# A second square per chunk taken in halves, its GpSimd work rearranged, and a VectorE order turned round, in a fused attention and two-layer kernel on one core

## The reference

```
x  = softmax(q k^T / sqrt(128)) k            # 768 pooled keys
h1 = x @ w_in1;  g1 = relu(h1)**2;  x2 = g1 @ w_out1          # 2048 wide
h  = x2 @ w_in2                                               # 2048 wide
g2 = (a0 + a1 h + a2 h^2 + a3 h^3) / (1 + |b0||h| + |b1|h^2 + 1e-6)
out = g2 @ w_out2
```

## Time and profile before

| | |
|---|---|
| time, median of 3 runs | 1517.82 us (1517.7 to 1518.0) |
| time of the profiled execution | 1517.89 us |
| its span | 1515.9 us |
| PE busy | 1483.7 us (98%) |
| DVE busy | 1445.2 us (95%) |
| ACT busy | 1378.8 us (91%) |
| POOL busy | 1248.3 us (82%) |
| granted TensorE clock | full throughout |

### The profile page before, as it was taken

The page is one execution under the profiler, slowest core; times in us unless marked ns, Lnnn a source line. Parts: engine busy times, 40 slices in busy tenths (PEclk is TensorE's granted clock), DMA queues, the critical chain, the costliest instruction groups (busy, mean ns, idle before and its releaser), DMA issues.

```text
span 1515.9 us, 20584 instructions
## 1 busy us (share of the span) xinstructions
PE 1483.7 (98%) x5576; PEld 991.1 (65%) x5576; DVE 1445.2 (95%) x2549; ACT 1378.8 (91%) x2672; POOL 1248.3 (82%) x1225
## 2 busy tenths in 40 slices
PE   5999999999999999999999999999999999999988
PEld 4999999765666666666666666666666666666655
DVE  7888888889999999999999999999999999999998
ACT  3777777689999999999999999999999999999997
POOL 4544445359999999999999999999999999999897
PEclk9999999999999999999999999999999999999999
DMA  6200001000000000000000000000000000000000
GB/s 224 84 21 28 21 27 43 1 1 1 8 8 8 1 8 8 8 8 1 7 8 8 0 8 8 8 1 8 7 8 1 8 8 8 8 1 8 8 8 7
DMA packets 11518, 24.21 MB, mean 16 GB/s; under 512 B 1440, under 2 KB 2336, under 8 KB 11168
## 3 DMA queue, kind: packets, MB, share of 16 engines
q1 hardware_dynamic: 11424, 23.14, 4.5%
HBM read 16.85 MB, written 6.29 MB: 15 GB/s over the span
## 4 chain that ended last, share of the span: by engine, by line
PE 88%; DVE 5%; ACT 2%; POOL 2%; issue 1%; DMA 1%; SPq 0%; POOLq 0%; ACTq 0%; DVEq 0%
PE psum L937 19%; PE psum L974 18%; PE psum L801 11%; PE psum L800 11%; PE psum L802 11%; PE psum L889 6%; PE psum L852 6%; PE psum L874 4%; DVE tb L727 1%; DVE tb L736 1%; DVE tb L753 1%; DVE g1h L713 1%; DVE psum L741 1%; POOL tb L410 1%; DMA X<-kvT 1%
## 5 line engine op out<-in xcount | busy, mean ns | idle before, releaser
L412 POOL TENSOR_TENSOR wb<-wb,ub 128x512 f32<-128x512 f32 x384 | 496.4, 1293 | 29.4
L937 PE MATMUL psum<-tb,wout 128*128 128x512 f32 x736 | 375.8, 592 | 2.5 <-DVE tb L785 2.3
L974 PE MATMUL psum<-g,wout 128*128 128x512 f32 x690 | 352.4, 592 | 0.2 <-ACT x2f L528 0.2
L404 POOL TENSOR_SCALAR wb<-ub,babs 128x512 f32<-128x512 f32 x384 | 296.0, 771 | 35.5 <-ACT ub L550 30.3
L800 PE MATMUL psum<-x2h,win2h 128*128 128x512 f32 x384 | 283.3, 738 | 2.6 <-POOL x2l L397 2.5
L727 DVE SCALAR_TENSOR_TENSOR tb<-tb,ca,psum 128x512 f32<-128x512 f32 x364 | 267.8, 736 | 4.6 <-ACT psum L584 4.5
L736 DVE SCALAR_TENSOR_TENSOR tb<-tb,ca,psum 128x512 f32<-128x512 f32 x365 | 269.6, 739 | 0.0
L551 ACT ACTIVATE tb<-psum,ca 128x512 f32<-128x512 f32 x384 | 267.1, 696 | 0.0
L550 ACT ACTIVATE ub<-psum 128x512 f32<-128x512 f32 x384 | 233.0, 607 | 23.5 <-PE psum L802 23.5
L568 ACT ACTIVATE lnb<-wb 128x512 f32<-128x512 f32 x384 | 248.3, 647 | 5.2 <-POOL wb L412 4.8
L753 DVE SCALAR_TENSOR_TENSOR tb<-psum,tb 128x512 f32<-128x512 f32 x364 | 248.1, 682 | 2.6
(11 more groups left out here) (109 smaller groups left out, 2506.6 us busy)
## 6 DMA issues: line engine op xcount, KB each, us to landing
qraw<-qT SPq DMA_DIRECT2D x23, 256.0 KB, 2.6
outT<-osb SPq DMA_DIRECT2D x23, 256.0 KB, 2.0
X<-kvT SPq DMA_DIRECT2D x15, 384.0 KB, 7.7
wraw<-w_in SPq DMA_DIRECT2D x2, 1024.0 KB, 8.3
X<-kvT SPq DMA_DIRECT2D x2, 192.0 KB, 10.5
outT<-osb SPq DMA_DIRECT2D x2, 128.0 KB, 1.8
qraw<-qT SPq DMA_DIRECT2D x1, 192.0 KB, 10.2
wsr<-w_sr SPq DMA_DIRECT2D x1, 64.0 KB, 1.8
```

The costliest lines, as they stand in the source:

```text
L404: nc.gpsimd.tensor_scalar(w, u, babs[:, 1:2], babs[:, 0:1], ALU.mult, ALU.add).then_inc(v_rdy, 1)
L412: nc.gpsimd.tensor_tensor(w, w, u, ALU.mult).then_inc(w_rdy, 1)
L937: mm(ACC2, wout2[:, f, :], tb[:, t % T_RING, :], start=(f == 0), stop=(f == NF - 1))\
L974: mm(ACC1, wout1[:, f, :], g1[:, t % G_RING, :], start=(f == 0), stop=(f == NF - 1))\
```

## The change

Three edits. First, column 5 is halved as column 13 is, and GpSimd's x1h and x1l, which stood together at step 5, move to step 6 and to step 8. Second, both places that wait for a low part (the first `in2` of a chunk, and `out1` of a halved column) do the two passes that need only the high part first, and wait for the low part in front of the third. Third, VectorE does T3 in front of y in every step but those in which GpSimd made T2 for that T3 (step 11); the steps of the tail keep their order.

```diff
-        SPLIT_COLS = (13,)
+        SPLIT_COLS = (5, 13)
...
-                if s % NF == 5 and 1 <= s // NF < NCH - 1:
+                if s % NF == 6 and 1 <= s // NF < NCH - 1:
                     x1_high(s // NF + 1)
+                if s % NF == 8 and 1 <= s // NF < NCH - 1:
                     x1_low(s // NF + 1)
...
             for s in range(TAIL_S):
-                t = s - LAG - 2
-                (y, then T3)
+                if by_pool(s - LAG - 1):
+                    make_y(s - LAG - 2)
+                    make_t3(s - LAG - 1)
+                else:
+                    make_t3(s - LAG - 1)
+                    make_y(s - LAG - 2)
...
                     if t % NF == 0:
-                        pe.wait_ge(*((x2l0_rdy, 1) if c == 0 else (x2_rdy, c)))
+                        pe.wait_ge(x2h_rdy, c + 1)
...
-                    three(h2(t), win2h[:, f:f + P], win2l[:, f:f + P],
-                          x2h[:, c % 2, :], x2l[:, c % 2, :]).then_inc(h2_rdy, 1)
+                    mm(h2(t), win2h[:, f:f + P], x2h[:, c % 2, :], start=True, stop=False)
+                    mm(h2(t), win2l[:, f:f + P], x2h[:, c % 2, :], start=False, stop=False)
+                    if t % NF == 0:
+                        pe.wait_ge(*((x2l0_rdy, 1) if c == 0 else (x2_rdy, c)))
+                    mm(h2(t), win2h[:, f:f + P], x2l[:, c % 2, :], start=False, stop=True).then_inc(h2_rdy, 1)
...
                         pe.wait_ge(sqh_rdy, n + 1)
+                        mm(ACC1, wo1h[:, f, :], g1h[:, n % 2, :], start=(f == 0), stop=False)
+                        mm(ACC1, wo1l[:, f, :], g1h[:, n % 2, :], start=False, stop=False)
                         pe.wait_ge(sql_rdy, n + 1)
-                        three(ACC1, wo1h[:, f, :], wo1l[:, f, :], g1h[:, n % 2, :], g1l[:, n % 2, :],
-                              start=(f == 0), stop=(f == NF - 1)).then_inc(g1_used, 1)
+                        mm(ACC1, wo1h[:, f, :], g1l[:, n % 2, :], start=False, stop=(f == NF - 1)).then_inc(g1_used, 1)
```

More of the change, by code:

```diff
@@ L720, in _, with make_y @@
             nc.vector.tensor_tensor(x2l[:, 0, :], ACC1, x2h[:, 0, :].bitcast(F32), ALU.subtract).then_inc(x2l0_rdy, 1)
-            for s in range(TAIL_S):
-                t = s - LAG - 2
+            def make_y(t):
                 if in_b(t):
@@ L728, in _, with make_t3 @@
                                                    op0=ALU.add, op1=ALU.mult).then_inc(y_rdy, 1)
-                t = s - LAG - 1
+            def make_t3(t):
                 if in_b(t):
@@ L737, in _ @@
                                                    op0=ALU.add, op1=ALU.mult).then_inc(t3_rdy, 1)
+            for s in range(TAIL_S):
+                if by_pool(s - LAG - 1):
[4 more added lines that the diff above has]
+                    make_y(s - LAG - 2)
                 t = s - LAG - 2
```

## The result

The changed kernel takes 1526.31 us, median of 6 runs (1525.96 to 1526.91), against 1517.92 us for the kernel before beside it: ratio 1.0056, 95% interval 1.0043 to 1.0069. It is slower by 8.4 us. I had forecast slower by 4.6, with 1519.5 to 1525.0 us as the range of the likeliest case; the direction is right, the size is not, and the time lies above that range.

What follows compares the result with a forecast made beforehand. It took TensorE as the bound before, and a GpSimd and ScalarE loop of 49.82 us a chunk after. 1.5 (chunk 1) + 3.6 (chunks 2 to 22) - 0.5 (end) = +4.6 us: 1522.4; likeliest range 1519.5 to 1525.0.

Steps and rivals of the forecast that it cites:

- A loop of GpSimd's and ScalarE's work: GpSimd steps 5 to 14, then ScalarE step 15 to next step 5: 49.8 us a chunk, over TensorE's 49.49.
- the new halved column's 0.16 us: TensorE, second halved column in chunks 1 to 23: saves 0.16 us each, 3.7 us, bound becomes 49.49 a chunk.
- the first chunk adds 1.5 us: Chunk 1, L412 of step 14 at 358.1 instead of 356.16: 1.5 us late, between 0.5 and 1.9 possible.
- the logarithm of step 15: ScalarE, profile after: it waits for GpSimd's wb by some 0.5 us and more.
- 3.6: Chunks 2 to 22: the longer loop adds 21 x 0.17 = 3.6 us.
- - 0.5: At the end: TensorE trails by 0.47 us less (third pass), and chunk 23 has no x1 work.
- 49.82: 0.17 us a chunk more than before: Period of the GpSimd and ScalarE loop from chunk 2 on, with 0.1 either way for rounding.
- L404 of step 5 starts 0.70 us after L550 starts: Crossing from ScalarE's ub to GpSimd in step 5, counted as 0.7 us of the loop.
- from step 5 to step 14 it now never idles: GpSimd, each chunk: an unbroken 32.2 us from L404 of step 5 to the end of step 14's L412.
- VectorE's order and the split waits at nothing: VectorE's exchange of y and T3 costed at no gain or loss; split waits gain nothing in steady state.
- Rival A: The loop doesn't close and TensorE stays the bound, period 49.49: 1513.6 to 1514.1 us, chance 0.18.
- Rival C: GpSimd work dearer: g1l at step 5 slowed a tenth under VectorE adds 2.8 us, 1525; chance 0.05.

Runs made afterwards that it cites:

- the last four versions: Changed kernel with x1h at step 3, x1l at step 9 (1515.15 us); same with VectorE's order undone (1515.56), waits undone (1516.06), both undone (1515.97).
- the two placements that kept GpSimd's heavy steps apart: Changed kernel with x1h, x1l at steps 3 and 9: 1515.15 us; with columns 3 and 13 halved, x1h, x1l at steps 1 and 7: 1515.58.

## Why the prediction was right and wrong

**The mechanism holds, as far as it went.** A loop of GpSimd's and ScalarE's work closes above TensorE's bound, the new halved column's 0.16 us are given back, and the first chunk adds 1.5 us. Of the signs that I had named, these are there: GpSimd waits in front of L405 of step 5 and next to nowhere from there to step 14, the logarithm of step 9 waits 0.67 us for wb (I had said about 1), the first `in2` waits for x2l at its third pass (0.27), and VectorE waits more (0.50 for 0.18 at the place of the earlier trace rows). One is not: the logarithm of step 15 was to wait by some 0.5 us and more, and starts only 0.26 us later than it would without a wait (0.83 after L552 of its step, 908.23, instead of 0.57). ScalarE comes to it nearly as late as GpSimd does, because it had itself been held up in step 11. What I had also not foreseen is that TensorE is stopped by x2f and by the copy of the output sums, both ScalarE's.

**The sum, term by term.** Forecast 1.5 + 3.6 - 0.5 = 4.6 us. Measured on the spans, the first x2l is 367.8 - 366.3 = 1.5 late (right to the tenth), and step by step the way forecast: L413 of step 14 of chunk 1 starts at 358.0, for which I had 358.1. The 21 periods of 49.98 - 49.65 = 0.33 are 6.9. The last period, 0.2 shorter than before, and what lies behind the last x2l, 0.6 longer, together add 0.4, where I had taken off 0.5. That makes 8.8. No run shows the 0.5: with the split waits the part behind the last x2l is not shorter.

The mis-sized term is the period, "49.82: 0.17 us a chunk more than before": it is 49.98, and 0.33 more. Two errors in it show in the chunk above.
- "L404 of step 5 starts 0.70 us after L550 starts". It starts 0.83 after (925.95 to 926.78). The instruction itself had become longer, 0.73 instead of 0.60, with the engine's start-to-start times unchanged.
- "from step 5 to step 14 it now never idles". GpSimd waits 0.13 us in step 13, for ub of 901.58. The longest loop is not the one that I added up: it leaves GpSimd at step 10 (wb of 895.63), runs over ScalarE to step 13, and comes back to GpSimd for steps 13 and 14.

The other spacings, as measured, are some 0.1 us shorter than my sum. So the loop with a single stretch on GpSimd is 30.81 + 1.33 + 16.89 + 0.83 = 49.86, close to the forecast, its two deviations nearly cancelling; the 0.13 us of the way over ScalarE make it 49.99 in this chunk. The step that failed is thus that the loop of GpSimd 5 to 14 and ScalarE 15 to 5 is the longest one. The same omission, of loops with two stretches, made the run with x1 at step 5 a miss.

Multiplied by 21, an error of 0.16 in 49.8 (a third of a per cent) was 3.3 us of the 4.2 that the forecast fell short; I had allowed 0.1 either way.

**The other steps.** TensorE's saving of 0.16 a halved column: right, and in full once the loop is shortened (49.48). By the Trainium skill, FP8 and Floating Point Precision, TensorE Precision Notes, a true fp32 product is four passes, and three would by that estimate save a quarter of the fp32 matmul, some 0.2 us; here the measured row was the better guide. VectorE's order and the split waits at nothing in the changed kernel: undoing either leaves nine tenths of the loss, and the runs don't tell the 0.7 and 0.9 us from nothing. Rival A, TensorE as the bound, is not what this kernel does, but what it does with two instructions elsewhere. Rival C, a dearer g1l, fell: its duration is 1.29 us in the median after and 1.27 before.

What stays open: the 0.6 us behind the last x2l, and whether the small differences of under 0.1% between the last four versions are real.

## What to carry to other kernels

When several engines are each over 80% busy and wait for one another every few microseconds, ask of a change not only whether each engine's work still fits, but which loops of work run through more than one engine: add the start-to-start times along GpSimd where it is the slower and along ScalarE where that is, with each crossing, until one period has passed, and look at loops with more than one stretch on either engine. The longest of them is the period. Here a ScalarE instruction on it cost its full time and the same one beside it nothing, and the two placements that kept GpSimd's heavy steps apart ran at TensorE's bound. Before adding work for a small gain on the bounding engine, place it: the same work cost 8.4 us with x1h and x1l in steps 6 and 8 and gained 2.7 with them in steps 3 and 9.

## What was not expected of the hardware

A ScalarE instruction's duration grows while the engine never waits, and with it the moment when its result can be used. In the chunk shown, |h| of a 128x512 tile takes 0.59 us at 910.60, right after a wait, 0.66 at 917.21 and 0.73 at 925.95, with the distance from one start to the next unchanged (0.47 to 0.57 us by kind). GpSimd, which waits for it, started 0.70 us after its start in the kernel before and 0.83 after it here. The next wait sets it back: 0.59 again.

The run with both low-part waits in front happens to test this. There TensorE holds ScalarE up a little in step 4: |h| starts 0.63 us after the instruction before it, not 0.52. Its ACT, step 4 and step 5, and its POOL, step 5:

```profile
922.16 0.71 ACT L585 ACTIVATE psum<-lnb 128x512 f32<-128x512 f32 x1
922.79 0.60 ACT L551 ACTIVATE ub<-psum 128x512 f32<-128x512 f32 x1
...
925.91 0.60 ACT L551 ACTIVATE ub<-psum 128x512 f32<-128x512 f32 x1
```

```profile
926.62 0.77 POOL L405 TENSOR_SCALAR wb<-ub,babs 128x512 f32<-128x512 f32 x1 [0.45 <-ACT ub L551]
```

The duration in step 5 is 0.60 again and GpSimd starts 0.71 after it: the short wait and the shorter crossing nearly cancel, and the period hardly changes (49.94 without the last, for 49.98). In these traces, then, a price read from start to start is right for the engine itself and too low for whoever waits at the end of a long unbroken run. Why the duration grows is not shown.
